# First layers of two MLPs as seven block products instead of eight, in pairs of token tiles, with weights streamed from memory

## What is computed

```python
scores = (1/S) * z @ z.T                 # per batch, S = 3008, z has 64 columns
x  = u * (np.maximum(scores, 0)**2 @ v)  # attention without softmax
h  = x @ w_in                            # MLP 1: 256 -> 2048
x  = (h - np.tanh(h)) @ w_out            #        2048 -> 256
g  = 1 / (1 + np.exp(-(x @ w_gate)))     # MLP 2: 256 -> 1536, twice
y  = (g * (x @ w_val)) @ w_out2          #        1536 -> 256
```

## Time and profile before

| | us |
|---|---|
| median of 3 runs | 1643.39 |
| lowest and highest | 1643.16, 1643.51 |
| the profiled execution's own time | 1643.4 |
| its span, first to last instruction | 1641.3 |
| TensorE busy (matmuls) | 1631.9, 7176 matmuls |
| VectorE busy | 856.0 |
| ScalarE busy | 741.0 |

### The profile page before, as it was taken

How to read it: one execution, slowest core, us unless ns; L and a number is a source line. 1 busy time by engine, 2 the same in 40 slices (tenths; PEclk the granted TensorE clock), 3 DMA queues, 4 the chain that set the end, 5 groups by cost and what they waited for, 6 DMA issues and landing times.

```text
span 1641.3 us, 19048 instructions
## 1 busy us (share of the span) xinstructions
PE 1631.9 (99%) x7176; PEld 1349.6 (82%) x7176; DVE 856.0 (52%) x885; ACT 741.0 (45%) x886; POOL 0.2 (0%) x4
## 2 busy tenths in 40 slices
PE   8999999999999999999999999999999999999999
PEld 6888888888888888888888888988888888888888
DVE  8766679766667544444444444643333333333333
ACT  7555567555556444444444444533333333333333
POOL 0000000000000000000000000000000000000000
PEclk9999999999999999999999999999999999999999
DMA  4100013200003100000000000310000000000000
GB/s 128 46 25 25 26 44 95 71 26 25 15 25 102 54 26 25 25 25 25 25 25 15 23 23 26 95 34 21 25 25 25 13 13 25 25 25 23 13 1 23
DMA packets 27702, 55.84 MB, mean 34 GB/s; under 512 B 2064, under 2 KB 20496, under 8 KB 27664
## 3 DMA queue, kind: packets, MB, share of 16 engines
q1 hardware_dynamic: 27664, 55.32, 10.5%
HBM read 36.83 MB, written 18.48 MB: 34 GB/s over the span
## 4 chain that ended last, share of the span: by engine, by line
PE 99%; DVE 1%; ACT 0%; DMA 0%; issue 0%; DVEq 0%; ACTq 0%
PE acc L277 17%; PE acc L276 17%; PE acc L278 17%; PE hidden L276 13%; PE hidden L278 13%; PE hidden L277 13%; PE hidden L297 4%; PE hidden L298 4%; PE acc L337 0%; PE acc L338 0%; DVE part_lo L450 0%; DMA stage<-zT 0%; DVE region_z L450 0%; DVE full L484 0%; ACT first L401 0%; ACT x_out L443 0%
## 5 line engine op out<-in xcount | busy, mean ns | idle before, releaser
L450 DVE TENSOR_TENSOR part_lo<-full,part_hi 128x1020 fp32r<-128x1020 f32 (+4 forms) x384 | 380.8, 992 | 415.6 <-ACT part_hi L418 160.1
L276 PE MATMUL acc<-part_hi,region_vh 128*128 128x510 f32 (+1 forms) x648 | 251.9, 389 | 0.8 <-DVE part_lo L450 0.8
L277 PE MATMUL acc<-part_lo,region_vh 128*128 128x510 f32 (+1 forms) x648 | 252.1, 389 | 0.0
L278 PE MATMUL acc<-part_hi,region_vl 128*128 128x510 f32 (+1 forms) x648 | 251.2, 388 | 0.0
L415 ACT ACTIVATE part_hi<-first 128x1020 fp32r<-128x1020 f32 (+1 forms) x144 | 150.1, 1043 | 207.0 <-PE acc L278 193.5
L490 DVE TENSOR_TENSOR full<-hidden,first 128x510 f32<-128x510 f32 (+1 forms) x144 | 98.0, 680 | 246.6 <-ACT first L409 246.6
L409 ACT ACTIVATE first<-hidden 128x510 f32<-128x510 f32 (+1 forms) x144 | 85.0, 590 | 266.7 <-PE hidden L278 266.7
L418 ACT ACTIVATE part_hi<-full 128x1020 fp32r<-128x1020 f32 (+1 forms) x96 | 100.1, 1043 | 169.0 <-PE acc L278 163.7
L484 DVE TENSOR_TENSOR full<-first 128x1020 f32<-128x1020 f32 (+1 forms) x144 | 172.2, 1196 | 1.4 <-ACT first L401 1.0
L487 DVE TENSOR_TENSOR full<-hidden,first 128x1020 f32<-128x1020 f32 (+1 forms) x96 | 115.4, 1202 | 109.2 <-ACT first L405 109.0
L405 ACT ACTIVATE first<-hidden 128x1020 f32<-128x1020 f32 (+1 forms) x96 | 96.8, 1008 | 128.9 <-PE hidden L278 128.9
(11 more groups left out here) (66 smaller groups left out, 2515.9 us busy)
## 6 DMA issues: line engine op xcount, KB each, us to landing
x_in<-xs SPq DMA_DIRECT2D x22, 510.0 KB, 4.0
xs<-x_out SPq DMA_DIRECT2D x21, 510.0 KB, 3.4
stage<-vP SPq DMA_DIRECT2D x24, 256.0 KB, 2.7
yT<-x_out SPq DMA_DIRECT2D x11, 510.0 KB, 3.2
u_in<-uT SPq DMA_DIRECT2D x10, 510.0 KB, 4.5
stage<-w SPq DMA_DIRECT2D x12, 384.0 KB, 3.0
stage<-w SPq DMA_DIRECT2D x8, 512.0 KB, 3.7
stage<-zT SPq DMA_DIRECT2D x12, 256.0 KB, 2.6
```

Of the source, the lines that this page charges most:

```text
L276: pe.matmul(dst, hi, mov_hi, start=start, stop=False)
L277: pe.matmul(dst, hi, mov_lo, start=False, stop=False)
L278: return pe.matmul(dst, lo, mov_hi, start=False, stop=stop)
L450: return ve.tensor_tensor(dst, whole, hi.bitcast(F32), ALU.subtract)
```

## The change

Tokens are now cut for the two MLPs into 6 pairs of tiles, 2 x 512 tokens but for the last pair (2 x 448). A unit of work is 2 feature chunks (256 hidden features) for the 2 tiles of a pair: 48 units in MLP 1 and 36 in MLP 2 (6 pairs x 8, 6 pairs x 6). The first layer of a unit is a product of a 2x2 block matrix of weights (chunk x channel half) with a 2x2 block matrix of x (channel half x tile), which takes 8 block products; Strassen's scheme in Winograd's form takes 7, of sums of the blocks. Each is made in split precision, three matmuls. One such set of seven is called a group; MLP 1 has one group per unit, MLP 2 two (gate and value, `s` = 0 and 1). The sums of x are made once per pair (`sum_x`, four subtractions, and seven splits), those of the weights once per unit in the attention stage, whence the split weights are written to memory (`ready`) and read back for every unit into one of three slots in turn (`load_slot`). The attention stage is as before with tiles of 512 (448), and all loops are unrolled.

```diff
-TOK = 510
...
+TOK = 512
...
+            def product(n, s, i):
...
+                bank = (CHAIN[group_of(n, s) % 2], BANK2, BANK7)[(0, 1, 2, 0, 0, 0, 2)[i]]
...
+                three(hidden[:, bank, 0:w], *weights, *x, i < 3, True).then_inc(s_prod, 1)
+
+            def products_begin(n, s):
...
+                product(n, s, 0)
+                if g > 0:
+                    pe.wait_ge(s_add, 3 * (g - 1) + 1)
+                product(n, s, 1)
...
+                    pe.wait_ge(s_add, 3 * (g - 1) + 3)
+                product(n, s, 2)
+                pe.wait_ge(s_snap, 3 * g + 1)
+                product(n, s, 3)
+
+            def products_middle(n, s):
+                pe.wait_ge(s_snap, 3 * group_of(n, s) + 2)
+                product(n, s, 4)
+
+            def products_end(n, s):
+                g = group_of(n, s)
+                pe.wait_ge(s_snap, 3 * g + 3)
+                product(n, s, 5)
+                pe.wait_ge(s_add, 3 * g + 2)
+                product(n, s, 6)
...
+            for n in range(1, NB):
+                products_begin(n, 0)
+                second(n - 1, 0)
+                products_middle(n, 0)
+                second(n - 1, 1)
+                products_end(n, 0)
+                second(n - 1, 2)
+                second(n - 1, 3)
+            for n in range(NB, NU):
+                for s in range(2):
+                    products_begin(n, s)
+                    second(n - 1, 2 * s)
+                    products_middle(n, s)
+                    second(n - 1, 2 * s + 1)
+                    products_end(n, s)
+            for b in range(4):
+                second(NU - 1, b)
...
+            def snapshot(n, s, i):
+
+                g, w = group_of(n, s), pair_width(pair_of(n))
+                act.wait_ge(s_prod, 7 * g + (1, 4, 5)[i])
+                act.activation(snap[:, g % 2, i, 0:w], hidden[:, CHAIN[g % 2], 0:w],
+                               ACT.Copy).then_inc(s_snap, 1)
+
+            def high(n, half):
...
+                act.wait_ge(s_g, 3 * n + (1, 3)[half])
...
+            def evacuate(q, tile):
+
+                w = pair_width(q)
+                act.wait_ge(s_out, 4 * first_unit(q + 1) - tile)
+                act.wait_ge(s_store, stores(q))
+                act.activation(x_out[:, :, tile, 0:w], acc[:, 2 * tile:2 * tile + 2, 0:w],
                                ACT.Copy).then_inc(s_evac, 1)
+
...
+            for n in range(NB, NU):
+                q, u, w = pair_of(n), unit_of(n), pair_width(pair_of(n))
+                g = group_of(n, 0)
+                snapshot(n, 0, 0)
+                high(n - 1, 1)
+                snapshot(n, 0, 1)
+                snapshot(n, 0, 2)
+                act.wait_ge(s_add, 3 * g + 2)
+                act.activation(t[:, 0:2, 0:w], t[:, 0:2, 0:w], ACT.Sigmoid).then_inc(s_t, 1)
+                act.wait_ge(s_prod, 7 * g + 6)
+                act.activation(t[:, 2, 0:w], hidden[:, CHAIN[g % 2], 0:w],
+                               ACT.Sigmoid).then_inc(s_t, 1)
+                snapshot(n, 1, 0)
+                act.wait_ge(s_add, 3 * g + 3)
+                act.activation(t[:, 3, 0:w], t[:, 3, 0:w], ACT.Sigmoid).then_inc(s_t, 1)
+                if q + 1 < NPAIR and 2 <= u < 5:
+                    split_x(q + 1, 2 * u - 4)
+                    split_x(q + 1, 2 * u - 3)
+                if q + 1 < NPAIR and u == 5:
+                    split_x(q + 1, 6)
+                snapshot(n, 1, 1)
+                snapshot(n, 1, 2)
+                if u == 0:
+                    evacuate(q - 1, 1)
+                    evacuate(q - 1, 0)
+                high(n, 0)
+            high(NU - 1, 1)
+            w = pair_width(NPAIR - 1)
...
+            def combine(n, s, i, dst):
+
+                g, w = group_of(n, s), pair_width(pair_of(n))
+                ve.wait_ge(s_snap, 3 * g + (1, 3, 2)[i])
+                ve.wait_ge(s_prod, 7 * g + (2, 3, 7)[i])
+                ve.tensor_tensor(dst, hidden[:, (BANK2, BANK7, BANK7)[i], 0:w],
+                                 snap[:, g % 2, (0, 2, 1)[i], 0:w], ALU.add).then_inc(s_add, 1)
+
+            def low(n, half):
...
+                ve.wait_ge(s_hi, 2 * n + half + 1)
+                minus(part_lo[:, b, 0:w], h[:, n % 2, b, 0:w],
+                      part_hi[:, b, 0:w]).then_inc(s_lo, 1)
...
+            for n in range(NB, NU):
+                q, u, w = pair_of(n), unit_of(n), pair_width(pair_of(n))
+                hn = h[:, n % 2]
+                combine(n, 0, 0, t[:, 0, 0:w])
+                low(n - 1, 1)
+                combine(n, 0, 1, t[:, 1, 0:w])
+                combine(n, 0, 2, t[:, 3, 0:w])
+                combine(n, 1, 0, hn[:, 0, 0:w])
+                if q + 1 < NPAIR and u < 2:
+                    sum_x(q + 1, 2 * u)
+                    sum_x(q + 1, 2 * u + 1)
+                if q + 1 < NPAIR and 2 <= u < 5:
+                    split_x(q + 1, 2 * u - 4)
+                    split_x(q + 1, 2 * u - 3)
+                if q + 1 < NPAIR and u == 5:
+                    split_x(q + 1, 6)
+                combine(n, 1, 1, hn[:, 1, 0:w])
+                ve.wait_ge(s_t, 3 * n + 1)
+                ve.wait_ge(s_add, 3 * group_of(n, 1) + 2)
+                ve.tensor_tensor(hn[:, 0:2, 0:w], hn[:, 0:2, 0:w], t[:, 0:2, 0:w],
+                                 ALU.mult).then_inc(s_g, 1)
+                combine(n, 1, 2, hn[:, 3, 0:w])
+                low(n, 0)
+                ve.wait_ge(s_t, 3 * n + 2)
+                ve.wait_ge(s_prod, 7 * group_of(n, 1) + 6)
+                ve.tensor_tensor(hn[:, 2, 0:w], hidden[:, CHAIN[1], 0:w], t[:, 2, 0:w],
+                                 ALU.mult).then_inc(s_g, 1)
+                ve.wait_ge(s_t, 3 * n + 3)
+                ve.wait_ge(s_add, 3 * group_of(n, 1) + 3)
+                ve.tensor_tensor(hn[:, 3, 0:w], hn[:, 3, 0:w], t[:, 3, 0:w],
+                                 ALU.mult).then_inc(s_g, 1)
+            low(NU - 1, 1)
...
+            def load_slot(n):
...
+                elif n == 2:
+                    sp.wait_ge(s_attn, NSTEP)
+                else:
+                    sp.wait_ge(s_out, 4 * (n - NSLOT + 1))
+                sp.dma_start(slot[n % NSLOT][:, 0:WUNIT[la]].bitcast(F32),
+                             ready[la][u]).then_inc(s_slot[n % NSLOT], 16)
```

More of the change, by code:

```diff
@@ L14 @@
 DH = DIM // P
-TPB = 6
-TOK = 510
+ALL = BATCH * SEQ
+TOK = 512
+TPB = -(-SEQ // TOK)
 NT = BATCH * TPB
-ALL = BATCH * SEQ
 KCH = -(-SEQ // P)
 SEQP = KCH * P
+STEPS = KCH // 2
+NSTEP = NT * STEPS
 ZP = 6
@@ L272, in _ @@
+            load_slot(1)
+            store_tile(NT - 1)
+            for n in range(NU):
+                q, u = pair_of(n), unit_of(n)
+                if u == 0 and q + 1 < NPAIR:
+                    load_x(q + 1)
+                if u == 1 and q > 0:
+                    store_pair(q - 1)
+                if n + 2 < NU:
+                    load_slot(n + 2)
+            store_pair(NPAIR - 1)
+            sp.wait_ge(s_store, stores(NPAIR))
         @block.tensor
         def _(pe):
-            def three(dst, hi, lo, mov_hi, mov_lo, start, stop):
-                pe.matmul(dst, hi, mov_hi, start=start, stop=False)
-                pe.matmul(dst, hi, mov_lo, start=False, stop=False)
-                return pe.matmul(dst, lo, mov_hi, start=False, stop=stop)
@@ L340, in O @@
-                        if ph == "A":
-                            w = [v[:, 2 * p + c, half] for v in (vh, vl)]
-                        elif ph == "B":
-                            w = [w1_pair(p)[:, s, c, DIM + d * P:DIM + (d + 1) * P]
-                                 for s in range(2)]
-                        else:
-                            w = [w2_chunk(p)[:, s, 2 * DIM + d * P:2 * DIM + (d + 1) * P]
-                                 for s in range(2)]
-                        last = three(dst, *w, hi, lo, start, stop)
@@ L349, in O @@
-                        if at == LAST_TILE and stop and d < DH - 1:
-                            last.then_inc(s_part, 1)
-                last.then_inc(s_o, 1)
-            def tile(ph, T, at):
-                for p in range(STEPS[ph]):
-                    q = p + LAG
-                    if q < STEPS[ph]:
-                        H(ph, T, at, q)
-                    elif at < LAST_TILE:
-                        H(phase_of(at + 1), T + 1, at + 1, q - STEPS[ph])
-                    O(ph, T, at, p)
@@ L363, in _ @@
-            for p in range(LAG):
-                H("A", 0, 0, p)
-            over_tiles(pe, tile)
+                        dst = acc[:, T % 2 * DH + d, 0:w]
+                        if 2 * p + c == KCH - 1:
+                            pe.matmul(dst, vh[:, KCH - 1, half], x_hi, start=False, stop=False,
+                                      skip_group_check=True)
+                            last = pe.matmul(dst, vl[:, KCH - 1, half], x_hi, start=False,
+                                             stop=True, skip_group_check=True)
+                        else:
```

(11 more changed lines are left out.)

788 lines of the change are left out of this document (472 added, 316 removed).

## The result

The changed kernel takes 1593.06 us (median of 4 runs, 1592.39 to 1593.95) against 1643.36 (1643.16 to 1643.51) beside it: a ratio of 0.9694, 95% interval 0.9678 to 0.9711. Forecast was 1628, range 1601 to 1656. It is 35 us faster than forecast and lies outside the range. The profiled execution took 1593.95 with a span of 1592.2.

The account below looks back on a forecast made before the run. The prediction took TensorE, busy 99% of the span, as the bound: 1641.3 - 81.6 for fewer matmuls + 43 + 2.5 + 4 + 3.5 + 6.6 + 1.5 + 4 + 1 = 1625.8 us span, forecast 1628, range 1601 to 1656.

Parts of the forecast that it names:

- 512 tokens cost 231.5 ns: TensorE's matmul slot at 512 tokens, from the line through 406 (184.8 ns) and 510 tokens, 0.441 ns per token.
- The stop in MLP 2: TensorE stands still 1.21 us per unit at the fifth product, 35 places, +43 us.
- the walk: Summed chain over ScalarE and VectorE between fifth products in MLP 2: 8.15 us against 6.94 of TensorE's work.
- The just-met waits: Two further MLP 2 waits met with 0.0 to 0.1 us to spare; 0 to 7.5 us, taken as +4.
- MLP 1's pair starts: Evacuations hold ScalarE and delay the fourth product in the first unit after a pair: 0.7 us, five pairs, +3.5.
- The seam: Attention to MLP 1: gate by u delays combine and `low`, third slot's weights land late; +6.6 us in all.
- The table load: Between MLP 1 and 2, one load of 1.28 us in a walk without slack: +1.5 us.
- The tail: Last unit's `second` waits for both `low`, 2.2 us, then a larger evacuation and store: +4 us.
- B: Rival: the stops are absent because hardware starts the chain's operations earlier; 1577, or up to 1600 us; chance 0.14.
- A: Rival: worse handovers, a 1.62 us stop per MLP 2 unit, slower than before, about 1650 us; chance 0.20.
- C: Rival: every MLP 2 stop sends the clock to its lower level, +81, about 1709 us; chance 0.05.
- D: Rival: weight transfers bind, +13 us in each of 12 pairs or more, 1780 us and up; chance 0.04.

Follow-up runs that it names:

- experiment 3: The changed kernel with tiles of 510 tokens, rows packed, instead of 512: 1619.23 us, ratio 0.9854.
- experiment 4: The changed kernel with two swaps in MLP 2: second snapshot ahead of `high` on ScalarE, second combine ahead of `low` on VectorE: 1547.33 us.
- experiment 8: experiment 4 with two more moves: at MLP 1 pair starts one evacuation into the second unit, at the seam VectorE's gating by u behind the second combination: 1542.97 us.

## Why the prediction was wrong

The step that failed is "512 tokens cost 231.5 ns". It extends the line through 406 and 510 by two tokens, and both points of that line are packed rows. As such the line is right: with rows 520 apart, every second one off the 64 bytes, 512 columns do take 231.2 ns. But packed rows of 512 lie 2048 bytes apart and all start at a multiple of 64, and then a slot is 226.8. Which of the two properties does it was not separated. What it weighs, by the prediction's own terms: the attention, costed at 0, won 7.7 us (its 2280 matmuls take 513.0 us, for 520.7); MLP 1 has 1800 slots of 512 at 4.6 ns less, 8.3 us; MLP 2 1980 at 4.9 less, 9.8. Together 25.8 us. Experiment 3 takes the layout away and has 26.2, if not of quite the same parts: its slots of 510 are 231.5 ns, about 1 more than in the kernel before, and its stops 0.15 us shorter each. The width was priced by its length alone.

The other terms, forecast against the trace:

- The matmuls' count: 6816, right. The 448 wide slots: 203.3 forecast, 203.8 in the mean.
- The stop in MLP 2, 1.21 us and 43 in all: the walk of 8.15 us is right to a few hundredths. With 30 slots of 0.2267 it leaves 8.15 - 6.80 = 1.35, and 1.31 was measured, 45.5 in all; experiment 4 gives 45.7. A faster slot only makes TensorE wait longer in a loop that it does not bound (1.16 us with the slots of experiment 3), so 2.5 of the 26 us were lost again here.
- The just-met waits, 4 us: 0.2. Besides the one stop no two matmuls of a unit in MLP 2 start over 0.30 us apart but for one distance at the start of the narrow pair (0.34), so the 2.5 for the evacuations are gone too.
- MLP 1's pair starts, 3.5: four of 0.48 and one of 0.2, 2.1. The walk had 0.7 each with five.
- The seam, 6.6: its gaps are 3.4 in all. VectorE's gate by u did hold up the combination (1.4 and 0.9 lost), but the third slot's weights came in time. They were issued 13.3 us after the first product, as forecast, but landed 7.7 us later and not 14, 1.9 us ahead of the product that needs them. The Trainium skill (DMA: Bandwidth & Descriptors, section Bandwidth) states 341 GB/s for 1 MB; at that rate 2304 KB take an estimated 6.9 us, to which the prediction's 7 to 8 is near. From the durations of the same table (6.15 us for 1 MB and 79.0 for 16 MB, without the issue), the estimate is 12 us. The 8.7 of the trace lies between the two, so the page did not decide it; the slope of two small transfers was too dear with 13.5.
- The table load 1.5: 0. It comes at 1006.0 us, and no gap of TensorE follows it. The 0.3 that was lost at this step is the wait for the first 2304 KB, which the prediction had put at nothing. The weights' preparation in the attention 1: 0 (442 matmuls to 100 us from 100 to 200).
- The tail 4: about 5.7. The pause is 2.3 as forecast (less the 0.3 of before), the slow slots add 1.5 (about 0.8 of it a loss, by experiment 8), and from the last matmul to the end it is 5.6 us for 3.4.

These sum to -25.8 + 2.5 - 3.8 - 2.5 - 1.4 - 3.2 - 1.2 - 1 + 1.7 = -34.7. The median lies 35 us under the forecast and the profiled span, from which the terms are read, 33.6 us, so about 1 us is not accounted for.

Of the rivals, B (no stops, 1577 to 1600) would have had the time right by the wrong reason: the stops are all there, and the time alone could not have told. A is out, since the handovers were as walked. C did not happen in MLP 2: 35 stops of 1.3 us and the granted clock stayed at 1.00 from 1036 to 1472. The Trainium skill (TensorE: Matmul & The Clock Gate, section A second HAM failure mode: psum-queue depth-cycling) warns of such a pattern of short pauses between groups; with 1.3 us in 16.3 the trace does not show it. D is out, with 8.7 us of transfer in a unit of 16.3. Of the signs that were to prove a step wrong, the slots of 231 ns failed; a transfer behind a gap and a clock below 1.00 came once each, and weigh 0.3 and about 0.8 us.

The largest saving was not in the forecast at all: the stop was found and priced in the walk, and one look further, at which of the two operations in ScalarE's queue is wanted first, gives 46 us for two exchanged lines.

## What to carry to other kernels

Price a change of tile width by how its rows lie (spacing and start) as well as by how long they are, and take both points of a line from rows laid out like the new one. Where the diff changes the width and the algorithm, cost them apart: here 26 to 31 of 50 us came from the former. In a loop bound by a chain over ScalarE and VectorE, walk the chain once with each queue's order as written and once with the operation for which TensorE waits moved up: `high`, whose result was wanted 27 matmuls later, stood ahead of a 0.6 us snapshot that released the next product.
